# Attention, mixture of experts and feed-forward in one kernel: first weights loaded and split in other iterations, chunk 3 of q and k issued ahead of v, the choice of experts spread over iterations, late gate sums ahead of the scores

## What is computed

```
scores = scale * q @ k^T, only where 0 <= row - col < 64      # q, k, v: 4 x 8 x 576 x 64
x = softmax(scores) @ v, as 2304 x 512                        # 18 tiles of 128 tokens
noisy = x @ w_gate + log1p(exp(x @ w_noise)) * noise          # 2304 x 8
for the two largest of noisy per token: weight w_k, expert e_k
x2 = sum_k w_k * relu(x @ w1[e_k]) @ w2[e_k]                  # w1: 8 x 512 x 1024, w2: 8 x 1024 x 512
h = x2 @ w_in;  out = (h * clip(h + 3, 0, 6) / 6) @ w_out     # 2048 wide
```

## Time and profile before

| | us |
|---|---|
| median of 3 runs | 1028.84 (1027.41 to 1032.24) |
| profiled execution | 1028.74 |
| its span | 1027.0 |
| PE busy | 996.8 (97%) |
| DVE busy | 417.9 (41%) |
| ACT busy | 229.6 (22%) |
| POOL busy | 427.6 (42%) |
| mean granted TensorE clock | 0.988 of full |

### The profile page before, as it was taken

How to read it: one execution, slowest core, us unless ns; L and a number is a source line. 1 busy time by engine, 2 the same in 40 slices (tenths; PEclk the granted TensorE clock), 3 DMA queues, 4 the chain that set the end, 5 groups by cost and what they waited for, 6 DMA issues and landing times.

```text
span 1027.0 us, 17976 instructions
## 1 busy us (share of the span) xinstructions
PE 996.8 (97%) x7108; PEld 886.1 (86%) x7108; DVE 417.9 (41%) x879; ACT 229.6 (22%) x537; POOL 427.6 (42%) x333
## 2 busy tenths in 40 slices
PE   7988879999999999999999999999999999999998
PEld 6766668999999999999989888999999999999997
DVE  3568754323222221222222246545535445454433
ACT  4656621211111111111111122111111111111111
POOL 3467854995664919184673928300101001000000
PEclk9989989999999999999999999999999999999999
DMA  9899676855362616244341334110101011100000
GB/s 156 176 216 244 186 255 215 273 166 194 104 215 64 205 71 201 97 147 172 101 166 63 123 122 157 50 44 21 42 31 41 20 46 38 39 1 1 31 1 32
DMA packets 125542, 116.17 MB, mean 113 GB/s; under 512 B 64800, under 2 KB 92960, under 8 KB 125472
## 3 DMA queue, kind: packets, MB, share of 16 engines
q1 hardware_dynamic: 106368, 75.36, 26.5%
q10 hardware_dynamic: 13344, 20.98, 5.9%
q0 software_dynamic: 5760, 18.88, 5.6%
HBM read 76.13 MB, written 39.06 MB: 112 GB/s over the span
## 4 chain that ended last, share of the span: by engine, by line
PE 89%; DMA 3%; DVE 3%; SPq 2%; POOL 1%; ACT 1%; issue 1%; DVEq 0%; POOLq 0%; ACTq 0%
PE PS L1556 21%; PE PS L1572 21%; PE PS L1692 19%; PE PS L1676 19%; PE PS L1540 2%; DMA k_later<-in_k_dram 1%; PE PS L1365 1%; SPq L467 1%; PE PS L1441 1%; PE PS L1617 1%; PE PS L1420 1%; PE PS L1404 1%; POOL x_sorted L683 1%; SPq L477 1%; DMA k_raw<-in_k_dram 1%
## 5 line engine op out<-in xcount | busy, mean ns | idle before, releaser
L1572 PE MATMUL PS<-W,hs_room 128*128 128x512 f32 x960 | 245.6, 399 | 0.0
L1556 PE MATMUL PS<-xs,W 128*128 128x256 f32 (+1 forms) x1536 | 244.2, 309 | 0.0
L1556 PEld LDWEIGHTS PS<-xs,W 128*128 128x128 f32 x1536 | 234.6, 189 | 10.6 <-issue 0.3
L1692 PE MATMUL PS<-W,gs 128*128 128x512 f32 x864 | 217.0, 395 | 0.9 <-DVE gs L1296 0.9
L1676 PE MATMUL PS<-x2s,W 128*128 128x384 f32 x1152 | 216.6, 337 | 0.0
L655 POOL TENSOR_TENSOR W<-stage,ones_f 128x1024 fp32r<-128x1024 f32 (+1 forms) x100 | 147.3, 1483 | 153.2 <-PE PS L1572 137.1
L1676 PEld LDWEIGHTS PS<-x2s,W 128*128 128x128 f32 x1152 | 201.3, 188 | 7.2
L1572 PEld LDWEIGHTS PS<-W,hs_room 128*128 128x128 f32 x960 | 174.6, 188 | 33.2
L1692 PEld LDWEIGHTS PS<-W,gs 128*128 128x128 f32 x864 | 161.2, 188 | 31.8 <-issue 1.6
L663 POOL TENSOR_TENSOR W<-stage,W 128x1024 fp32r<-128x1024 f32 (+1 forms) x100 | 185.5, 1866 | 5.8
L1147 DVE SCALAR_TENSOR_TENSOR hs_room<-PS,hs_room 128x256 fp32r<-128x256 f32 (+1 forms) x128 | 62.9, 491 | 293.7 <-ACT hs_room L860 293.7
(11 more groups left out here) (133 smaller groups left out, 571.1 us busy)
## 6 DMA issues: line engine op xcount, KB each, us to landing
stage<-in_moe_w_dram SPq DMA_DIRECT2D x64, 512.0 KB, 4.0
y_sorted<-y_sb ACTq DMA_DIRECT2D x40, 256.0 KB, 3.1
x_in<-x_sorted ACTq DMA_DIRECT2D x38, 256.0 KB, 4.7
x_sorted<-zeros SPq DMA_DIRECT2D x7, 1280.0 KB, 7.6
vD<-in_v_dram SPq DMA_DIRECT2D x72, 64.0 KB, 2.7
out_dram<-o_sb SPq DMA_DIRECT2D x18, 256.0 KB, 2.0
stage<-in_moe_w_in_dram SPq DMA_DIRECT2D x8, 512.0 KB, 3.8
stage<-in_moe_w_out_dram SPq DMA_DIRECT2D x8, 512.0 KB, 3.7
```

The lines of the kernel that those rows point to most:

```text
L1556: last = nc.tensor.matmul(HP_[:, c % 2, 0:n], W[:, par, 0, b, at:at + P], xs[part][:, a, kd, :], start=start, stop=(kd == KD - 1 and (a, b ...
L1572: last = nc.tensor.matmul(Y[:, first + t, :], hs[:, c % 2, a, t * P:(t + 1) * P], W[:, par, 1, b, c * DM:(c + 1) * DM], start=(c == 0 and ...
L1692: last = nc.tensor.matmul(OP[:, tt, :], gs[:, c % 2, a, tt * P:(tt + 1) * P], W[:, 1, c // FC, b, at:at + DM], start=(c == 0 and (a, b) == ...
```

## The change

Chunk 3 of q and k is issued ahead of v1, the gate weights and v2, and v0 ahead of all these. Expert 0's weights are loaded at T=3, 4, 7, 9, 10, 14, 15, 16 and split at T=4, 7, 8, 11, 12; the last three chunks are split after the scatters of lot 2 and the `keep_x` up to tile 16. The fill of x_sorted goes from T=6 to T=5. Parts 0 to 4 of the choice are placed anew: for lot 1 parts 0, 1 and 2 at T=9, 3 and 4 at T=10 (before: 0 and 1 at T=9, 2, 3 and 4 at T=10). At T=15 and 16 gate_sum stands between the masks and the products of the scores, and DVE's move_lg ahead of row_max.

```diff
-    FIRST_AT = (2, 3, 4, 5, 7, 8, 10, 11)
-    SPLIT_AT = (3, 4, 5, 6, 8, 9, 12, 13)
+    FIRST_AT = (3, 4, 7, 9, 10, 14, 15, 16)
+    SPLIT_AT = (4, 7, 8, 11, 12)
+    ZERO_X_AT = 5
...
             load_qk(1, both)
             load_qk(2, both)
+            load_v(0)
+            load_qk(3, both)
+            load_v(1)
             for n, w in enumerate((wg, wn)):
                 sp.dma_start(wgn[:, :, n * E:(n + 1) * E], w.rearrange("(k p) e -> p k e", p=P)).then_inc(s_small, 16)
-            for t in range(3):
-                load_v(t)
+            load_v(2)
             for T in range(TILES):
                 iteration(T)
-                if T == 0:
-                    load_qk(3, both)
                 if T == 0:
                     load_v(3)
...
-                if T == 6:
+                if T == ZERO_X_AT:
...
             for t in range(max(SCATTER_AT) - 1, TILES - 1):
                 keep_x(t)
+            for c in range(len(SPLIT_AT), SCH):
+                first_there(c)
+                split_hi(0, c, PIECES)
+                split_lo(0, c, c + 1, PIECES)
             keep_x(TILES - 1)
...
             for T in range(TILES + 1):
-                for after, part in ((4, 1), (5, 2)):
-                    for n in due(T, after):
-                        route(n, part)
+                for n in due(T, 5):
+                    route(n, 2)
...
                     move_first(item_at(T))
+                for n in due(T, 3):
+                    route(n, 0)
                 if T < TILES:
                     move_pt(T, 0)
                 if T >= 2:
                     move_xt(T - 2)
                 for n in due(T, 3):
-                    route(n, 0)
+                    route(n, 1)
...
             for T in range(TILES):
+                if T >= LOOP[1]:
+                    move_lg(T - 3)
                 if T + 1 < TILES:
                     row_max(T + 1)
-                if T >= 3:
+                if 3 <= T < LOOP[1]:
                     move_lg(T - 3)
+                for n in due(T, 3):
+                    route(n, 0)
                 if item_at(T) is not None:
                     move_second(item_at(T))
-                for after, parts in ((RANKS_AFTER, (5, 6)), (3, (0,)), (4, (2, 3))):
+                for after, parts in ((RANKS_AFTER, (5, 6)), (3, (1,)), (4, (3,))):
...
-                for after, part in ((3, 1), (4, 4), (5, 7)):
+                for after, part in ((3, 2), (4, 4), (5, 7)):
...
+                if between is not None:
+                    between()
...
-                if T + 1 < TILES:
-                    scores(T + 1, i)
-                if T >= 3:
-                    gate_sum(T - 3, i)
+                if LOOP[1] <= T < TILES - 1:
+                    scores(T + 1, i, lambda: gate_sum(T - 3))
+                else:
+                    if T + 1 < TILES:
+                        scores(T + 1, i)
+                    if T >= 3:
+                        gate_sum(T - 3, i)
```

More of the change, by code:

```diff
@@ L1366, in turn_qk, with scores @@
                 last.then_inc(ld_full, 1)
-            def scores(T, i=None):
+            def scores(T, i=None, between=None):
                 pe.wait_ge(ld_act, up(items_before(T), i))
```

## The result

The changed kernel took **1036.38 us** (median of 20 runs, 1031.47 to 1059.57) against 1028.84 (20 runs, 1025.58 to 1036.32): ratio 1.0064, 95% interval 1.004 to 1.0088. It is slower, outside the range and on the other side of my forecast of 1025.0. What has to be explained is not one number: the profiled execution is one of the longest (1057.22 us, span 1055.5), and in three of four later groups with this very kernel it took 1025.8 to 1026.6 us. I read the profile for what differs in kind first, and set it beside other profiles of the same kernel further down; the profile of r_after2, an execution of 1044.91 us, has the same at 174 us.

The account below looks back on a forecast made before the run. Until 62 us SP's queue was taken to set the pace, then DVE's choice of experts and POOL's scatters. +0.3 - 1.0 - 1.5 - 1.5 = -3.7 from 1028.74 gave 1025.0 us; range 1017.5 to 1029.5.

Parts of the forecast that it names:

- part 5: Three splits after lot 2's scatters keep POOL for 15.6 us; cost 0, bounds 0 and +3 us.
- Cover: that idle time: POOL's 9.55 us of idle time before lot 4's slots come was to cover the late splits.
- three later loads share the DMAs: Three later weight loads share the DMAs with the scatters, 1.5 us each, within the bound of part 5.
- Part 1: Chunk 3's loads ahead: T=3's stall goes, some 3.5 us, but PE waits that much longer at T=7; worth nothing.
- Part 2: Weight loads and x_sorted fill moved: k of chunk 5 lands 0.3 us later, bounds -1.5 to +2.9.
- rival one: SP's queue really comes ahead, idle time at T=7 shrinks: 1014.8 us, or half, 1019.9; chance 0.22.
- rival two: The fill holds k of chunk 5 at T=7, landing later than 66.0 us: 1030.2 us; chance 0.10.
- Part 3: Choices spread and splits moved: T=10 falls 1.0 us to 5.8, T=11 falls 1.5 us to 7.4.
- rival three: The port lock moves to T=11, which keeps 8.93 us; T=12 waits 1.5 for g_parts: 1028.0 us; chance 0.13.
- Part 4: gate_sum moved at T=15 and 16: lot 2's slots come 1.5 us sooner, bounds 0 to -2.6.
- what would show it: Signs listed for right or wrong, such as slot_cur of lot 2 at 117 us, or PE idle in expert 0.

Follow-up runs that it names:

- r_after2: The changed kernel with no edit, run again on chip 7: 1042.3 us (1030.85 to 1058.18), ratio 1.0053.
- r_pool7: The changed kernel with seven copies on POOL ahead of the three late splits, chip 6: 1030.49 us, ratio 1.0026.
- r_latefill: The kernel before with SP's last two y_sorted fills issued after the wait for pads_ready, chip 7: 1034.86 us, ratio 1.0056.
- r_force: The changed kernel with SP's last two y_sorted fills held back until DVE's choices are ranked, chip 10: 1031.92 us, ratio 1.003.
- r_wonly: The kernel before with only the weight schedule changed (loads, splits, x_sorted fill), chip 10: 1026.35 us, ratio 0.9975.
- r_after: The changed kernel with no edit, run again on chip 10: 1026.58 us, ratio 0.998.
- r_after3: The changed kernel with no edit, run again on chip 2: 1026.53 us, ratio 0.9987.
- r_after4: The changed kernel with no edit, run again on chip 10: 1025.82 us, ratio 0.9973.
- r_guard: The changed kernel, but POOL waits for DVE's places in y_sorted before it splits expert 1's weights, chip 2: 1026.9 us, ratio 0.9979.
- r_fills: The changed kernel with SP's last two y_sorted fills issued ahead of expert 1's first four weight loads, chip 10: 1027.07 us, ratio 0.9984.
- r_fills2: The same edit of the changed kernel as r_fills, run on chip 2: 1024.93 us, ratio 0.9969.
- group 1: First set of follow-up runs, on chip 10, with the kernel before at 1028.14 us; it holds r_after, r_fills and r_wonly.
- r_pool7fills: r_pool7 with SP's last two y_sorted fills ahead of expert 1's stage loads, chip 6: 1027.55 us, ratio 1.0001.

## Why the prediction was wrong

**The step that failed is part 5**, "Cost 0", with "Cover: that idle time". The cover was real but I spent it against one profile. Laid out: POOL had 8.25 us of idle time ahead of lot 3 and 9.55 ahead of lot 4; 15.6 us of splits took the first and part of the second, and left 5.01 in a calm execution (I had said about 3; lot 3's first scatter came at 150.06, 3.3 us later than before, where I had some 10) and 0.48 in the profile on record, where lot 2's slots came at 122.95. With the cover gone I had written +3 as a bound; r_pool7 lies 4.2 us above the mean of the calm controls (1030.49 against 1026.3), and where ACT stands as well the times go up to 1059.57. And I named only lot 3's scatters as waiting for the splits. SP's queue waits too: expert 1's stage loads need the stage buffers that the late splits free, and the last two y_sorted fills stand behind them, 13 us later than before. These fills among lot 4's scatters cost 5.1 us (r_latefill) and 6.1 us (r_force). My own "three later loads share the DMAs" counted the wrong transfers.

**Part 1:** T=3's stall went, 3.7 us shorter, but the new order is not shown to be what did it. T=3 takes 5.97 us in r_wonly too, which has the old order, and 6.38 in r_latefill, whose attention is that of before. In both T=4 starts at 37.0 or 36.9, as in the changed kernel (37.02), against 38.81 in the one profile I had. The stall wanders between T=3, T=5 and T=7 from one execution to the next: T=5 took 5.75 in that profile and 6.57 to 11.20 in the five of the changed kernel. PE waited at T=7 for 3.70 us on record, not 7.5, having got there 1.0 us sooner and not 3.5.

**Part 2:** within its bounds. k of chunk 5 landed at 60.62, 1.4 us sooner than before where I had 0.3 later. Neither rival one nor two came (before 60, after 66). My price of the fill, 266 GB/s, is not a fill's rate in general: from 153.0 to 153.4 us in r_after the only packets are 272 of a y_sorted fill, of 512 bytes each, and they go at 348 GB/s, near the 355 that I took for the stage loads. With that rate the landing would have been forecast 0.7 us sooner, nearer to what came.

**Part 3:** T=11 right in size (7.4 forecast, 7.70 in the changed kernel on every chip, no wait for g_parts at T=12, so rival three is out). T=10 wrong: 5.8 forecast, 6.87 and, in r_after, 6.71. The four steps of old part 2 were to lie "where DVE waits for the next scores". In r_after there is no such wait: they end right at row_max, and logits are 0.79 us late behind it. onep did fall, to 0.16 us on record and 0.58 in r_after, but two of the four steps took 0.60 and 0.62 in both. The gains come from the new places of the splits: r_wonly has them without the spread and takes 5.83 at T=10 and 7.69 at T=11. The spread adds nothing at T=11 and takes back 0.9 at T=10.

**Part 4:** the size is right, the reason is not shown. From the start of T=15 to lot 2's slots it took 7.07 us before and 5.60 in every profile of the changed kernel, the one on record too: 1.5 sooner, as forecast. But r_wonly, whose gate sums stand where they stood, has 5.60 as well. Seen from the start of the span the slots were to come at about 117 (120.78 less 3.7); in calm profiles they came at 117.89 (r_after), 119.17 (r_after3) and 118.36 (r_after4), on record at 122.95, since there T=8 and T=12 took 1.6 and 1.7 us more than in r_after (7.74 against 6.18, 7.66 against 5.95), and T=14 0.3.

**The sum** of -3.7 us came out as -2.1 (mean ratio 0.998 of the three calm controls, of 1028.8), so without the failed step the forecast would have stood: 1026.3 on average of the three, 1.3 above 1025.0. That it comes as near as it does is in part luck: the weight schedule alone gives 0.9975, so most of what I gave to the choices and the gates belongs to the splits' new places, which I priced only within part 3.

**The chances:** 0.05 for slower was too little because the one thing of that sign that happened, a margin used up, was tied to rival two and not counted by itself. The list of what would show it did hold the right line: PE idle in expert 0, part 5.

**What stays open.** Why T=8 and T=12 are long and ACT waits for something unseen on chip 7 and on record, and not elsewhere, with the same instructions; since chip 7 was used once, chip and hour cannot be told apart, and the chip of the executions on record is not known. In the long iterations row_max starts 0.6 us (T=8) and 1.1 us (T=12) later than in r_after, and PE stands 0.3 to 0.4 us in times_v with no releaser that the profile shows. What ACT waits for is open too. The one packet of an instruction queue in this stretch is no candidate: in twelve profiles it starts 1.2 to 5.2 us after DVE has begun its tables, early or late with them, and in the two with the long stand it comes 2.3 to 2.4 us after ACT has gone on. That DVE's small operations beside POOL's splits cost PE two waits is read from the profile on record; no edit tested it, for no group with r_guard showed the long times. r_guard and r_fills on chip 7, beside r_after, would be the test. That the change turns a late loop into 7.5 and 12.6 us more by the medians (6.6 and 5.5 by the ratios), when the kernel before bears it (1029.75 on chip 7), is measured. That it does so by the lost idle time and the late fills is shown in part: their prices, 4.2 and 5.1 to 6.1 us, come from edits; the long stand of ACT was never made by one.

**A better version?** r_fills2 has the lowest time of all (1024.93), but its gain on the control of its group (1026.53) lies within the spread, the same edit stood 0.5 above its control in group 1 (1027.07 and 1026.58), and on chip 7 it was not run. By r_pool7fills it is still the one to keep: no cost shows where all is calm, and it gives back 2.9 us where POOL is late.

## What to carry to other kernels

Idle time that covers a move is a margin against variation too: read how much is left after the move, not only whether it is enough in the one profile at hand. When a step is put off, follow every queue that waits for the buffers it frees to the last transfer behind them, not just the one that is needed next. And where an unchanged kernel's runs agree on every chip, a changed one's need not: take controls in each group before a cause is named, and look for the signs of a slow group in the profiles of the kernels that are not slow. Where the gain of a step is read as right because an iteration has fallen, look at that iteration in a run that lacks the step.

## What was not expected of the hardware

- The changed kernel took 1025.8 to 1026.6 us in three groups on two chips and 1042.3 on a third (1030.85 to 1058.18), with the kernel before between 1028.1 and 1029.9 on all of them. Kernels with and without the change have the same signs on that third chip (T=8 at 6.8 to 7.9 us for 5.8 to 6.4), and only the changed one pays for them.
- ACT can stand 9 to 11 us in the middle of a stage (it ran at 176.52 and 174.50) with its input in place (the matmuls of L1576 that it reads had ended by 165.7) and no releaser in the profile. Three profiles on the same chip have 1.7 us of it, two of them with neither late splits nor late fills. In r_pool7 at 348 GB/s it did not happen, so full DMA engines alone don't do it.
- A DVE operation on 128x8 elements took 1.8 to 2.2 us beside POOL's splits of 1.9 and 2.4 us, against 0.17 without; operations in a chain pay it again and again (nine of 1.8 to 2.5 us between 178 and 200 us). Behind each of PE's waits of 5 to 8 us in this stretch its clock was granted at the lower level (0.50 from 178 to 182 us), which cost another 6.0 us.
- A fill of zeros is not free traffic late in a stage: two of them among scatters cost 5.1 and 6.1 us of 1029, for 2.3 us of issuing on SP.
